# One fused attention and two-MLP kernel on one core: first loads cut and reordered, weight and value splits moved, y stores issued by another engine

## Chip, core and metric

The kernel runs on one core of one Trainium2 chip. The metric is the device time of one execution in microseconds (us). The engines of a core run side by side and meet only at semaphores: TensorE (PE, matmuls and their weight loads), VectorE (DVE), ScalarE (ACT), GpSimd (POOL) and SyncE (SP, which here only issues DMAs). ACT can issue DMAs too. Each engine takes its instructions strictly in the order in which they are written.

## What is computed

Chunked attention with memory keys, then two MLPs on its output; everything in float32.

```python
for c in range(nc):                      # 24 chunks of 32 queries, 16 keys left, 8 right, 8 memory keys
    scores = scale * np.matmul(q_c, k_full.transpose(0, 1, 3, 2))
    scores = scores - np.max(scores, axis=-1, keepdims=True)
    a = np.exp(scores)
    a = a / (np.sum(a, axis=-1, keepdims=True) + 1e-09)
    out[:, :, c_start:c_end] = np.matmul(a, v_full)
x = out.transpose(0, 2, 1, 3).reshape(3072, 512)
h = x @ w_in                             # 512 x 2048
g = np.maximum(h, 0.0) + alpha * np.minimum(h, 0.0)
y = g @ w_out                            # 2048 x 512
return ((y @ w_a) * (y @ w_b)) @ w_out2  # 512 x 1536, 1536 x 512
```

## The kernel before

**Precision by splits.** Matmuls run on operands that are split in two: `hi` is the value rounded to a short float32 form (an ACT copy, helpers `hi_*`), `lo` is the value minus `hi` (a subtraction on POOL or DVE, helpers `lo_*`, `split_*`). A product is three matmuls: hi*hi, hi*lo, lo*hi (lines 585 to 587).

**Tiles.** The 3072 tokens are 8 tiles of 384 tokens. A tile has 8 attention heads; one head of one tile is a *unit*, and comes as one packed array of 128 rows x 1152 columns (K, then Q, each with its 64 rows written twice, then V in columns V0 = 896 and up): 576 KB. Two units make a pair, and a pair gives one quarter of the tile's `x`.

**Prologue (heads 0 to 8).** Units 0 to 10 are loaded into `u_early` by SP. For each head PE computes scores from unsplit data (`score_early`, line 621, into the one bank `s_ps`), DVE masks them and takes the maximum (`softmax_max`, line 1157), ACT takes the exponentials (`exps`, line 897, four per head), DVE inverts the sums, POOL normalises (line 538), PE transposes (line 636), DVE copies the transpose (`copy_pt`, line 1179), and per half pair PE multiplies with V (`mix_early`, line 647), ACT and DVE split the result into `x_hi` (line 915) and `x_lo` (line 1193). Between these stand steps that tile 0 will need: the splits of four weight blocks (`hi_w` on ACT line 886, `lo_w` on POOL line 532; `w_in_prologue(u)` says behind which head's exponentials), of the V of units 8 and 9 (`hi_v` line 872, `lo_v` line 506) and of K and Q of unit 9 (`hi_kq` line 863, `lo_kq` lines 517 and 522). `keep_busy(n)` (line 611) issues n matmuls whose result nobody reads. The first four weight blocks are staged in two slots `w_raw`, so that blocks 2 and 3 are loaded only when blocks 0 and 1 have been split.

**Tiles.** In tile t, for j = 0 to 15, PE computes `up` (12 matmuls, into `h_ps`) for j and `down` (12 matmuls, into four banks) for j - 1, and between them the attention steps of tile t + 1. In tile 0 the weights are split on the way: `up(0, j)` waits for weight block 2j, `down` for block 2j + 1. `up(0, 0)` waits for `x_lo` quarter by quarter; in its middle stand two `keep_busy` matmuls and the last pair's `mix_early`. POOL does per unit `lo_v`, `lo_kq` and, in tile 0, two `lo_w` per j. At the start of tile t + 1 ACT and DVE empty the four banks of tile t into `y_stage`, and ACT issues the store of it to `y_dram` (`store_y`, line 943).

**Second part.** Products of the second MLP (lines 591 to 593) and the last projection (lines 826 to 828), whose 24 outputs ACT copies to `o_stage` (line 1083) and SP stores (line 462).

## Time and profile before

| | us |
|---|---|
| three runs | 1212.30, 1212.31, 1212.92 |
| median | 1212.31 |
| the profiled execution | 1212.38 |
| span of its instructions | 1210.6 |
| PE busy | 1199.2 |
| DVE, ACT, POOL busy | 724.5, 569.0, 256.1 |
| TensorE clock granted, mean | 1.0 of full |

The span is the time from the first to the last instruction or transfer of the profiled execution; 1.8 us of its time lie around it. All times below are us from the start of the span. A row of the timeline has start, duration, engine and line, operation, what it writes and reads, how many were merged, and in brackets how long the engine had been idle and what released it. "PEld" is PE's weight load; "SPq" and "ACTq" are those engines' sequencers issuing DMAs.

### The profile page before, as it was taken

What the parts mean: (1) busy time and instruction counts of PE and PEld (TensorE: products, weight loads), DVE (VectorE), ACT (ScalarE), POOL (GpSimd) and SP (SyncE); (2) the same over time, 40 slices, a digit from 0 to 9 for tenths busy, and PEclk for the clock granted to TensorE, in tenths of its full rate; (3) what the DMA queues carried; (4) which work ended last, traced back from release to release, by engine and by line L of the source; (5) the groups of instructions that cost most, each with busy time, mean ns of one, the idle gap of its engine ahead of it and who ended that gap; (6) DMA issues with size and microseconds to landing.
All of it is one profiled execution on the core that took longest, in us unless ns stands there. A gap on an engine that the chain in (4) does not pass through costs nothing.

```text
span 1210.6 us, 19095 instructions
## 1 busy us (share of the span) xinstructions
PE 1199.2 (99%) x6616; PEld 1094.4 (90%) x6618; DVE 724.5 (60%) x1772; ACT 569.0 (47%) x1404; POOL 256.1 (21%) x234
## 2 busy tenths in 40 slices
PE   8999999999999999999999999999999999999998
PEld 5899999999999999999999888888888888888887
DVE  5777666666666666666555476854475644565421
ACT  6766454545454545454323454543444443444322
POOL 4886232323232323232035000000000000000000
PEclk9999999999999999999999999999999999999999
DMA  7452212112112121121110512022111121111000
GB/s 279 144 164 87 84 60 85 59 59 84 59 58 85 59 84 59 58 85 40 45 53 35 198 37 70 35 96 70 44 35 70 42 98 61 44 40 66 1 35 35
DMA packets 27619, 87.89 MB, mean 73 GB/s; under 512 B 2720, under 2 KB 6816, under 8 KB 25248
## 3 DMA queue, kind: packets, MB, share of 16 engines
q1 hardware_dynamic: 23328, 80.76, 19.9%
q10 hardware_dynamic: 4224, 6.29, 1.4%
q8 instruction: 36, 0.59, 0.2%
q14 instruction: 31, 0.25, 0.1%
HBM read 74.46 MB, written 12.58 MB: 72 GB/s over the span
## 4 chain that ended last, share of the span: by engine, by line
PE 96%; DVE 2%; ACT 1%; DMA 1%; issue 1%; POOL 0%; ACTq 0%; DVEq 0%; POOLq 0%
PE bank L585 16%; PE bank L587 15%; PE bank L586 15%; PE bank L592 9%; PE bank L593 9%; PE bank L591 9%; PE bank L827 5%; PE bank L826 5%; PE bank L828 5%; PE bank L604 2%; PE bank L636 1%; PE bank L603 1%; DMA w_raw<-w 1%; DVE g_lo L1213 0%; PE bank L611 0%
## 5 line engine op out<-in xcount | busy, mean ns | idle before, releaser
L592 PE MATMUL bank<-yc,ws 128*128 128x512 f32 x504 | 196.1, 389 | 0.0
L593 PE MATMUL bank<-yc,ws 128*128 128x512 f32 x504 | 196.1, 389 | 0.0
L591 PE MATMUL bank<-yc,ws 128*128 128x512 f32 x504 | 196.1, 389 | 0.0
L1203 DVE TENSOR_SCALAR g_neg<-bank,al 128x384 f32<-128x384 f32 x128 | 79.0, 617 | 173.8 <-PE bank L587 173.7
L926 ACT ACTIVATE g_hi<-g_raw 128x384 fp32r<-128x384 f32 x128 | 67.2, 525 | 120.3 <-DVE g_raw L1208 120.2
L897 ACT ACTIVATE prob<-prob,neg_max 96x128 f32<-96x128 f32 x220 | 85.7, 391 | 74.9 <-DVE neg_max L1157 74.9
L591 PEld LDWEIGHTS bank<-yc,ws 128*128 128x128 f32 x504 | 94.6, 188 | 19.7
L593 PEld LDWEIGHTS bank<-yc,ws 128*128 128x128 f32 x504 | 94.6, 188 | 19.6
L592 PEld LDWEIGHTS bank<-yc,ws 128*128 128x128 f32 x504 | 94.6, 188 | 19.6
L1402 DVE TENSOR_TENSOR p_split<-p_all,p_split 128x512 fp32r<-128x512 f32 x72 | 49.5, 691 | 93.5 <-ACT p_split L1077 93.4
L1077 ACT ACTIVATE p_split<-p_all 128x512 fp32r<-128x512 f32 x72 | 45.2, 631 | 110.3 <-PE bank L828 100.7
L522 POOL TENSOR_TENSOR k_lo<-u_raw,kq_hi 128x512 fp32r<-128x512 f32 x53 | 68.5, 1293 | 115.9 <-PE bank L604 115.3
L585 PE MATMUL bank<-g_hi,w_first 128*128 128x384 f32 x256 | 88.2, 345 | 0.7 <-DVE g_lo L1213 0.7
L585 PE MATMUL bank<-g_hi,w_later 128*128 128x384 f32 x256 | 88.0, 344 | 0.5 <-DVE g_lo L1213 0.5
L585 PE MATMUL bank<-x_hi,w_first 128*128 (+1 forms) x256 | 87.0, 340 | 1.2 <-DVE x_lo L1193 1.2
L1213 DVE TENSOR_TENSOR g_lo<-g_raw,g_hi 128x384 fp32r<-128x384 f32 x128 | 77.2, 603 | 16.3 <-ACT g_hi L926 12.7
L506 POOL TENSOR_TENSOR v_lo<-u_raw,v_hi 128x256 fp32r<-128x256 f32 x53 | 43.9, 829 | 201.1 <-ACT v_hi L872 201.1
L585 PE MATMUL bank<-x_hi,w_later 128*128 (+1 forms) x256 | 86.4, 338 | 0.0
L587 PE MATMUL bank<-g_hi,w_later 128*128 128x384 f32 x256 | 85.9, 335 | 0.0
L587 PE MATMUL bank<-g_hi,w_first 128*128 128x384 f32 x256 | 85.9, 335 | 0.0
L586 PE MATMUL bank<-g_lo,w_first 128*128 128x384 f32 x256 | 85.8, 335 | 0.0
L586 PE MATMUL bank<-g_lo,w_later 128*128 128x384 f32 x256 | 85.8, 335 | 0.0
(149 smaller groups left out, 3004.1 us busy)
## 6 DMA issues: line engine op xcount, KB each, us to landing
u_raw<-units SPq DMA_DIRECT2D x53, 576.0 KB, 3.7
wr<-w_ab SPq DMA_DIRECT2D x18, 1024.0 KB, 4.8
u_early<-units SPq DMA_DIRECT2D x11, 576.0 KB, 8.9
y_dram<-y_stage ACTq DMA_DIRECT2D x8, 768.0 KB, 4.1
out<-o_stage SPq DMA_DIRECT2D x24, 256.0 KB, 2.0
w_raw<-w SPq DMA_DIRECT2D x16, 256.0 KB, 2.9
y_stage<-w SPq DMA_DIRECT2D x16, 256.0 KB, 3.0
wr<-y_dram SPq DMA_DIRECT2D x8, 512.0 KB, 4.2
```

What stands on the lines that cost most here:

```text
L522: nc.gpsimd.tensor_tensor(k_lo[:, :], src[:, 0:Q0], kq_hi[:, b, 0:Q0].bitcast(F32), ALU.subtract).then_inc(k_lo_done, 1)
L585: nc.tensor.matmul(out_ap, w_hi, m_hi, start=first, stop=False)
L586: nc.tensor.matmul(out_ap, w_hi, m_lo, start=False, stop=False)
L587: return nc.tensor.matmul(out_ap, w_lo, m_hi, start=False, stop=last)
L591: nc.tensor.matmul(out_ap, w_hi, m_hi, start=first, stop=False, skip_group_check=True)
L592: nc.tensor.matmul(out_ap, w_hi, m_lo, start=False, stop=False, skip_group_check=True)
L593: return nc.tensor.matmul(out_ap, w_lo, m_hi, start=False, stop=True, skip_group_check=True)
L826: nc.tensor.matmul(r_ps[u % 2][:, :], hi, w[:, 0], start=g == order[0] and c == 0, stop=False)
L897: last = nc.scalar.activation(dst[:, i, :], src[:, i, :], ACT.Exp, bias=neg_max[:, b, i:i + 1], scale=-1.0, accum_out=row_sum[:, b, i, 0:1])
L926: nc.scalar.activation(g_hi[:, j % 2], g_raw[:, :], ACT.Copy).then_inc(g_hi_done, 1)
L1203: nc.vector.tensor_scalar(g_neg[:, :], h_ps[:, 0:TOK], 0.0, al[:, j:j + 1], ALU.min, ALU.mult)\
L1213: nc.vector.tensor_tensor(g_lo[:, j % 2], g_raw[:, :], g_hi[:, j % 2].bitcast(F32), ALU.subtract)\
```

## The change

Seven edits, all but the last two in the prologue.

1. Of unit 0 only 64 rows and columns 0 to 895 are loaded at first (224 KB), and the scores of head 0 contract over 64 rows with the whole scale; the V columns follow after unit 1 in a load of their own (128 KB).
2. The loads are in another order: weight blocks 0, 1 and 2 stand between units 1 and 4, alpha and block 3 behind unit 8. Each of the four blocks is loaded into the place of its own lower half (`w_first_raw`), so none waits for a slot.
3. The splits of weight blocks 0, 1, 2 follow heads 0, 1, 3 (were 0, 2, 5); block 3 and the V of units 8 and 9 and K, Q of unit 9 come behind the exponentials of head 8 on ACT, and on POOL behind the normalisation of head 8.
4. `keep_busy` has 8 for 10 matmuls at first, 2 for 3 ahead of transposes, and its two in the middle of `up(0, 0)` are gone.
5. The last pair's `mix_early` stands ahead of `up(0, 0)`, not in its middle.
6. The stores of `y` of tiles 0 to 5 are issued by SP, at the head of each pass of its loop, ahead of that tile's unit loads; those of tiles 6 and 7 stay on ACT.
7. The last output block is copied and stored in two halves of 256 columns: the first by SP, the second by ACT.

Core of the diff (declarations of the new semaphores and of `w_first_raw`, and the branches that pick them, are left out):

```diff
@@ sync
+            sp.dma_start(u_early[0:HEAD_DIM, 0, 0:V0], units[0][0:HEAD_DIM, 0:V0]).then_inc(first_loaded, 16)
+            load_early(1)
+            sp.dma_start(u_early[:, 0, V0:], units[0][:, V0:]).then_inc(early_loaded[0], 16)
+            load_w(0)
+            load_early(2)
+            load_w(1)
+            load_early(3)
+            load_w(2)
+            for u in range(4, HEADS + 1):
+                load_early(u)
+            sp.dma_start(al[:, :], alpha).then_inc(alpha_loaded, 16)
+            load_w(3)
...
+            def store_y(t):
+                sp.wait_ge(y_act_done, t + 1)
+                sp.wait_ge(y_dve_done, t + 1)
+                sp.dma_start(y_dram[:, :, bass.ds(t * TOK, TOK)], y_stage[:, :, :]).then_inc(y_stored, 16)
+
             with sp.Fori(1, TILES - 2) as t:
+                store_y(t - 1)
                 for c in range(HEADS):
                     load_unit((t + 1) * HEADS + (c + 4), c % 2)
+            store_y(TILES - 3)
@@ gpsimd
-            return {0: (0,), 2: (1,), 5: (2,), 8: (3,)}.get(u, ())
+            return {0: (0,), 1: (1,), 3: (2,)}.get(u, ())
...
-                if u == 4:
-                    lo_v(HEADS, HEADS)
-                if u == 6:
-                    lo_v(HEADS + 1, HEADS + 1)
-            pool.wait_ge(w_lo_done, W_PROLOGUE)
-            pool.wait_ge(v_lo_done, 2)
+            pool.wait_ge(prob_done, HEADS + 1)
             lo_kq(HEADS + 1, HEADS + 1)
+            lo_w(W_PROLOGUE - 1)
+            lo_v(HEADS, HEADS)
+            lo_v(HEADS + 1, HEADS + 1)
@@ tensor
-                    if first_tile and j == 0 and kt == 2:
-                        keep_busy(2)
-                        mix_early(PAIRS - 1, 0)
-                        mix_early(PAIRS - 1, 1)
...
-            keep_busy(10)
+            keep_busy(8)
...
-                        keep_busy(3)
+                        keep_busy(2)
...
+            mix_early(PAIRS - 1, 0)
+            mix_early(PAIRS - 1, 1)
             tile(0, 2)
@@ scalar
-                    if p == 0 and not first:
-                        store_y(t - 1)
...
-                if u == 3:
-                    hi_v(HEADS, HEADS)
-                if u == 5:
-                    hi_v(HEADS + 1, HEADS + 1)
-                if u == 7:
-                    hi_kq(HEADS + 1, HEADS + 1, 0)
             split_x(PAIRS - 2, 1, PAIRS - 2, 0, True)
+            hi_kq(HEADS + 1, HEADS + 1, 0)
             split_x(PAIRS - 1, 0, PAIRS - 1, 0, True)
             split_x(PAIRS - 1, 1, PAIRS - 1, 0, True)
+            hi_w(W_PROLOGUE - 1)
+            hi_v(HEADS, HEADS)
+            hi_v(HEADS + 1, HEADS + 1)
...
+                half = slice(0, MODEL if u < SUPERS * SUBS - 1 else MODEL // 2)
+                nc.scalar.activation(o_stage[:, u % 2, half], r_ps[u % 2][:, half], ACT.Copy).then_inc(o_done, 1)
...
+            nc.scalar.activation(o_stage[:, 1, MODEL // 2:], r_ps[1][:, MODEL // 2:], ACT.Copy).then_inc(last_copied, 1)
+            act.wait_ge(last_copied, 1)
+            act.dma_start(out[last_row:last_row + P, MODEL // 2:], o_stage[:, 1, MODEL // 2:]).then_inc(last_stored, 16)
```

On ACT, from the exponentials of head 3 (written to `y_stage`; even heads write `prob`) to those of head 7, the kernel before has:

```order
L897 ACTIVATE y_stage,row_sum<-y_stage,neg_max 96x128 x4
L872 ACTIVATE v_hi<-u_early 128x256
L897 ACTIVATE prob,row_sum<-y_stage,neg_max 96x128 x4
L915 ACTIVATE x_hi<-bank 64x192 x2
L897 ACTIVATE y_stage,row_sum<-y_stage,neg_max 96x128 x4
L915 ACTIVATE x_hi<-bank 64x192 x2
L886 ACTIVATE w_first<-w_raw 128x512
L872 ACTIVATE v_hi<-u_early 128x256
L897 ACTIVATE prob,row_sum<-y_stage,neg_max 96x128 x4
L915 ACTIVATE x_hi<-bank 64x192 x2
L897 ACTIVATE y_stage,row_sum<-y_stage,neg_max 96x128 x4
```

and the changed kernel:

```order
L930 ACTIVATE y_stage,row_sum<-y_stage,neg_max 96x128 x4
L919 ACTIVATE w_first<-w_first_raw 128x512
L930 ACTIVATE prob,row_sum<-y_stage,neg_max 96x128 x4
L948 ACTIVATE x_hi<-bank 64x192 x2
L930 ACTIVATE y_stage,row_sum<-y_stage,neg_max 96x128 x4
L948 ACTIVATE x_hi<-bank 64x192 x2
L930 ACTIVATE prob,row_sum<-y_stage,neg_max 96x128 x4
L948 ACTIVATE x_hi<-bank 64x192 x2
L930 ACTIVATE y_stage,row_sum<-y_stage,neg_max 96x128 x4
```

Both copies of V (`v_hi`) have left this stretch, and the weight block stands two heads earlier. Behind them, from head 7's split of `x` to the start of tile 0, the kernel before has on ACT:

```order
L915 ACTIVATE x_hi<-bank 64x192 x2
L863 ACTIVATE kq_hi<-u_early 128x896
L897 ACTIVATE prob,row_sum<-y_stage,neg_max 96x128 x4
L915 ACTIVATE x_hi<-bank 64x192 x2
L886 ACTIVATE w_first<-w_raw 128x512
L915 ACTIVATE x_hi<-bank 64x192 x6
L863 ACTIVATE kq_hi<-u_early 128x896
L872 ACTIVATE v_hi<-u_early 128x256
```

and the changed kernel:

```order
L948 ACTIVATE x_hi<-bank 64x192 x2
L930 ACTIVATE prob,row_sum<-y_stage,neg_max 96x128 x4
L948 ACTIVATE x_hi<-bank 64x192 x4
L893 ACTIVATE kq_hi<-u_early 128x896
L948 ACTIVATE x_hi<-bank 64x192 x4
L919 ACTIVATE w_first<-w_first_raw 128x512
L902 ACTIVATE v_hi<-u_early 128x256 x2
L893 ACTIVATE kq_hi<-u_early 128x896
L902 ACTIVATE v_hi<-u_early 128x256
```

The copy of K and Q of unit 9 went from ahead of head 8's exponentials to the middle of the last splits of `x`. On POOL, from the normalisation of head 6 (into `prob`) to the first weight blocks of tile 0, before:

```order
L538 TENSOR_TENSOR prob<-prob,inv_sum 96x512
L506 TENSOR_TENSOR v_lo<-u_early,v_hi 128x256
L538 TENSOR_TENSOR y_stage<-y_stage,inv_sum 96x512
L538 TENSOR_TENSOR prob<-prob,inv_sum 96x512
L532 TENSOR_TENSOR w_first<-w_raw,w_first 128x512
L517 TENSOR_TENSOR kq_hi<-u_early,kq_hi 64x384
L522 TENSOR_TENSOR k_lo<-u_early,kq_hi 128x512
L506 TENSOR_TENSOR v_lo<-u_early,v_hi 128x256
L517 TENSOR_TENSOR kq_hi<-u_early,kq_hi 64x384
L522 TENSOR_TENSOR k_lo<-u_early,kq_hi 128x512
L532 TENSOR_TENSOR w_first<-w_raw,w_first 128x512 x2
```

and changed:

```order
L569 TENSOR_TENSOR prob<-prob,inv_sum 96x512
L569 TENSOR_TENSOR y_stage<-y_stage,inv_sum 96x512
L569 TENSOR_TENSOR prob<-prob,inv_sum 96x512
L548 TENSOR_TENSOR kq_hi<-u_early,kq_hi 64x384
L553 TENSOR_TENSOR k_lo<-u_early,kq_hi 128x512
L563 TENSOR_TENSOR w_first<-w_first_raw,w_first 128x512
L537 TENSOR_TENSOR v_lo<-u_early,v_hi 128x256 x3
L548 TENSOR_TENSOR kq_hi<-u_early,kq_hi 64x384
L553 TENSOR_TENSOR k_lo<-u_early,kq_hi 128x512
L563 TENSOR_TENSOR w_first<-w_raw,w_first 128x512 x2
```

Two `v_lo` more stand between the last normalisation and the first weight blocks of tile 0 (the last row).

## Rows read from the trace of the kernel before

**Rows 1.** Page, part 1: busy time of each engine.

```profile
PE 1199.2 (99%) x6616; PEld 1094.4 (90%) x6618; DVE 724.5 (60%) x1772; ACT 569.0 (47%) x1404; POOL 256.1 (21%) x234
```

**Rows 2.** Timeline of ACT in the prologue: start, duration, engine, operation, idle.

```profile
14.26 0.40 ACT L897 ACTIVATE y_stage<-y_stage,neg_max 96x128 f32<-96x128 f32 x1
...
18.05 0.42 ACT L872 ACTIVATE v_hi<-u_early 128x256 fp32r<-128x256 f32 x1 [2.14 <-DMA u_early<-units]
...
18.37 0.39 ACT L897 ACTIVATE prob<-y_stage,neg_max 96x128 f32<-96x128 f32 x1
...
29.52 0.39 ACT L897 ACTIVATE prob<-y_stage,neg_max 96x128 f32<-96x128 f32 x1
...
30.97 0.19 ACT L897 ACTIVATION_READ_ACCUMULATOR prob<-y_stage,neg_max 96x1 f32 x1
```

**Rows 3.** Timeline of DVE: first maximum of head 6 and of head 7.

```profile
21.51 0.29 DVE L1157 CUSTOM_DVE_ANT_0 y_stage<-bank,mask 96x128 f32<-96x128 f32 x1
...
23.84 0.29 DVE L1157 CUSTOM_DVE_ANT_0 y_stage<-bank,mask 96x128 f32<-96x128 f32 x1
```

**Rows 4.** Timeline of the start: first load, first matmuls, first weight load of scores.

```profile
0.75 0.86 SPq L392 DMA_DIRECT2D u_early<-units  x2
...
0.79 4.42 PE L611 MATMUL bank<-const-bfloat16-1.0 128*128 128x512 bf16 x10 [0.79 <-PEq L1512]
...
4.96 1.20 PEld L621 LDWEIGHTS bank<-u_early 128*96 128x96 f32 x8 [0.66 <-DMA u_early<-units]
```

**Rows 5.** Page, part 6: loads, count, size of one, median us to landing.

```profile
u_raw<-units SPq DMA_DIRECT2D x53, 576.0 KB, 3.7
...
w_raw<-w SPq DMA_DIRECT2D x16, 256.0 KB, 2.9
```

**Rows 6.** Timeline: head 2's transpose; last mixes, splits of x, last quarter of up(0, 0).

```profile
15.59 0.55 PE L636 MATMUL bank<-ident,prob 96*128 96x96 f32 x4 [0.22 <-POOL prob L538]
...
32.09 1.46 PE L647 MATMUL bank<-pt_early,u_early 128*128 128x192 f32 x8
...
33.89 0.66 ACT L915 ACTIVATE x_hi<-bank 64x192 fp32r<-64x192 f32 x2
...
35.50 0.44 PE L585 MATMUL bank<-x_hi,w_first 128*128 128x384 f32 x1 [0.71 <-DVE x_lo L1193]
```

**Rows 7.** Timeline of POOL from head 8 on, and PE's start of up(0, 2).

```profile
32.63 1.27 POOL L532 TENSOR_TENSOR w_first<-w_raw,w_first 128x512 fp32r<-128x512 f32 x1
...
36.29 0.73 POOL L506 TENSOR_TENSOR v_lo<-u_early,v_hi 128x256 fp32r<-128x256 f32 x1
...
37.10 1.00 POOL L517 TENSOR_TENSOR kq_hi<-u_early,kq_hi 64x384 fp32r<-64x384 f32 x1
...
39.44 2.87 POOL L532 TENSOR_TENSOR w_first<-w_raw,w_first 128x512 fp32r<-128x512 f32 x2
44.58 2.54 POOL L532 TENSOR_TENSOR w_first<-y_stage,w_first 128x512 fp32r<-128x512 f32 x2 [2.28 <-ACT w_first L886]
...
42.17 0.33 PE L585 MATMUL bank<-x_hi,w_first 128*128 128x384 f32 x1
```

**Rows 8.** Timeline: y stores on ACT's queue, and what waits near them.

```profile
122.07 3.02 ACTq L943 DMA_DIRECT2D y_dram<-y_stage  x1
...
127.81 0.44 PE L585 MATMUL bank<-g_hi,w_first 128*128 128x384 f32 x1 [0.72 <-DVE g_lo L1213]
...
136.08 0.95 ACT L863 ACTIVATE kq_hi<-u_raw 128x896 fp32r<-128x896 f32 x1
...
607.27 0.56 ACTq L943 DMA_DIRECT2D y_dram<-y_stage  x1
...
611.37 0.53 ACT L926 ACTIVATE g_hi<-g_raw 128x384 fp32r<-128x384 f32 x1 [3.63 <-DVE g_raw L1208]
```

**Rows 9.** Timeline of the end: last output copy and its store.

```profile
1207.48 0.60 ACT L1083 ACTIVATE o_stage<-bank 128x512 f32<-128x512 f32 x1 [6.98 <-PE bank L828]
...
1208.11 0.33 SPq L462 DMA_DIRECT2D out<-o_stage  x1
```

More of the change, by code:

```diff
@@ L153, in attention_mlp_kernel @@
         x_ps, y_ps, z_ps, r_ps = (s_ps, pt_ps), (o_ps, h_ps), (bank[0], bank[1]), (bank[2], bank[3])
+        first_loaded = sem("first_loaded")
+        w_first_loaded = [sem(f"w_first_loaded{i}") for i in range(W_PROLOGUE)]
         early_loaded = [sem(f"early_loaded{i}") for i in range(EARLY)]
@@ L230, in attention_mlp_kernel @@
         o_done = sem("o_done")
+        last_copied = sem("last_copied")
+        last_stored = sem("last_stored")
         out_stored = [sem(f"out_stored{i}") for i in range(2)]
@@ L257, in stage_of @@
         def stage_of(n):
-            if W_PROLOGUE <= n < W1_UNITS:
-                return (n - W_PROLOGUE) % (W_STAGE + W_MORE)
-            return n % W_STAGE
+            return (n - W_PROLOGUE) % (W_STAGE + W_MORE)
         def w_stage(n):
+            if n < W_PROLOGUE:
+                return w_first_raw[:, n, 1]
             i = stage_of(n)
@@ L267, in before_in_stage @@
         def before_in_stage(n):
-            return [m for m in range(n) if stage_of(m) == stage_of(n)]
+            return [m for m in range(W_PROLOGUE, n) if stage_of(m) == stage_of(n)]
         def parity(t):
@@ L380, in load_w @@
             def load_w(n):
+                if n < W_PROLOGUE:
+                    sp.dma_start(w_stage(n), w1[n]).then_inc(w_first_loaded[n], 16)
+                    return
                 before = before_in_stage(n)
@@ L389, in load_w, with load_early @@
                 sp.dma_start(w_stage(n), w1[n]).then_inc(w_loaded[stage_of(n)], 16)
-            for u in range(EARLY):
+            def load_early(u):
                 sp.dma_start(u_early[:, u], units[u]).then_inc(early_loaded[u], 16)
-                if u == 1:
-                    sp.dma_start(al[:, :], alpha).then_inc(alpha_loaded, 16)
-                    load_w(0)
-                    load_w(1)
+            sp.dma_start(u_early[0:HEAD_DIM, 0, 0:V0], units[0][0:HEAD_DIM, 0:V0]).then_inc(first_loaded, 16)
[10 more added lines that the diff above has]
+            load_w(3)
+            for u in range(HEADS + 1, EARLY):
+                load_early(u)
             load_unit(EARLY, EARLY % 2)
-            for n in range(W_STAGE, W_PROLOGUE + W_STAGE + W_MORE):
+            for n in range(W_PROLOGUE, W_PROLOGUE + W_STAGE + W_MORE):
                 load_w(n)
@@ L461, in store_out @@
                 row = (u // SUBS) * TOK2 + rows_of(u % SUBS) * P
-                sp.dma_start(out[row:row + P, :], o_stage[:, u % 2]).then_inc(out_stored[u % 2], 16)
+                half = slice(0, MODEL if u < SUPERS * SUBS - 1 else MODEL // 2)
+                sp.dma_start(out[row:row + P, half], o_stage[:, u % 2, half]).then_inc(out_stored[u % 2], 16)
             sp.wait_ge(x_lo_done, UNITS)
@@ L486, in _ @@
                 sp.wait_ge(out_stored[i], 16 * SUPERS * SUBS // 2)
+            sp.wait_ge(last_stored, 16)
         @block.gpsimd
@@ L613, in score_early @@
             def score_early(u):
-                pe.wait_ge(early_loaded[u], 16)
+                rows = slice(0, P if u else HEAD_DIM)
+                pe.wait_ge(early_loaded[u] if u else first_loaded, 16)
                 if u:
@@ L618, in score_early @@
                 for i in range(BLOCKS):
-                    q = u_early[:, u, Q0 + i * QB:Q0 + (i + 1) * QB]
+                    q = u_early[rows, u, Q0 + i * QB:Q0 + (i + 1) * QB]
                     at = slice(i * KEYS, (i + 1) * KEYS)
-                    last = nc.tensor.matmul(s_ps[0:QB, at], q, u_early[:, u, at], start=True, stop=True)
+                    last = nc.tensor.matmul(s_ps[0:QB, at], q, u_early[rows, u, at], start=True, stop=True)
                 last.then_inc(scores, 1)
@@ L644, in mix_early @@
                     pe.wait_ge(x_lo_done, (g - 2) * 2 + half + 1)
+                if g == 0 and half == 0:
+                    pe.wait_ge(early_loaded[0], 16)
                 dst = half_bank(g, half, True)
@@ L880, in hi_w @@
             def hi_w(n):
-                act.wait_ge(w_loaded[stage_of(n)], 16 * (len(before_in_stage(n)) + 1))
+                if n < W_PROLOGUE:
+                    act.wait_ge(w_first_loaded[n], 16)
+                else:
+                    act.wait_ge(w_loaded[stage_of(n)], 16 * (len(before_in_stage(n)) + 1))
                 if n == EARLY_SLOTS:
@@ L1082, in empty_o @@
                     act.wait_ge(out_stored[u % 2], 16 * (u // 2))
-                nc.scalar.activation(o_stage[:, u % 2], r_ps[u % 2][:, :], ACT.Copy).then_inc(o_done, 1)
+                half = slice(0, MODEL if u < SUPERS * SUBS - 1 else MODEL // 2)
+                nc.scalar.activation(o_stage[:, u % 2, half], r_ps[u % 2][:, half], ACT.Copy).then_inc(o_done, 1)
             act.wait_ge(x_lo_done, UNITS)
```

10 lines of the change are left out of this document (4 added, 6 removed).

## Prediction, made before the changed kernel ran

> **What bounds the kernel now.** First the busy times: PE is busy 1199.2 us of the 1210.6 us span [rows 1], so only PE's idle time, some 11 us, can be won without less matmul work, and the change takes out only matmuls that nobody reads. The question is therefore where PE idles and whether a moved step opens or closes such a hole. The timeline then shows three places. The first is the prologue, up to the last quarter of up(0, 0) at 35.50 [rows 6]: PE works only in pieces there, and what ends last is the round score, maximum, exponentials, sum, normalise, transpose. The second is one hole of 0.72 us at 127.81 [rows 8]. The third is the end, where nothing but the copy and the store of the last block runs [rows 9]. In the other loop passes PE has no hole at the y stores, so no gain can be had there, only a loss. I work against the profiled execution, 1212.38 us with a span of 1210.6; the median of three, 1212.31, is the same within its scatter (1212.30 to 1212.92). About 0.2%, 2.4 us, is what a measurement of this kernel tells from no change.
>
> **Start of head 0.** Its first weight load is at 4.96, released by the load of unit 0, which SP issued at 0.75: 4.2 us [rows 4]. No row has a load of 224 KB; the nearest are 576 KB in 3.7 us and 256 KB in 2.9 us [rows 5], 0.8 us for 320 KB. The 352 KB fewer give 0.9, so it lands at about 4.05. PE's ten idle-filling matmuls take 4.42 us from 0.79 with their tail, their spacing about 0.43; eight of them end near 4.2. I take 4.25, so 0.7 us sooner. Bounds: 0 if a smaller load lands no sooner, 0.75 where the eight matmuls end. The order of the next loads does not take this back: units 1 to 3 have 0.35, 0.5 and 0.2 MB less ahead of them, units 4 to 8 the same bytes within 0.05 MB. From the landings of units 0 and 8 (4.96, 18.05, with 5.2 MB between them) a unit takes 1.5 us, so unit 4 lands near 12.1 and unit 8 near 18.1; the scores of a head start with the exponentials of the one before, now at 13.55 for head 4 and about 22.9 for head 8, so even the closest has 1.4 us.
> The Trainium skill (DMA: Bandwidth & Descriptors, Rules for kernel authors) advises against two transfers to disjoint partition halves, since both run on the same 16 DMA engines. Here the second 64 rows are not needed at all, but if the rule held for the one half as well, the 0.7 us would be gone and the sum 0.7 us smaller.
>
> **Pace of the heads.** Exponentials of head 3 start at 14.26, then ACT waits for unit 8's landing to copy its V at 18.05, and head 4 starts at 18.37 [rows 2], 1.9 us behind a pace of 2.2 to 2.3. A second loss lies before head 6, where ACT waits for weight block 2 and copies the V of unit 9, a third before head 8: the copy of K and Q of unit 9, 0.95 us as that at 136.08 [rows 8]. Head 8 starts at 29.52 and ends at 31.16 (30.97 + 0.19). With these gone, what is late next? DVE: between maximum of head 6 and of head 7 it works without a gap on maximum, inverse, copy of a transpose and x_lo, 23.84 - 21.51 = 2.33 us [rows 3]. ACT needs less, 1.55 for four exponentials and 0.66 for x_hi. So from head 3, now at 14.26 - 0.7 = 13.55, five steps of 2.33 give head 8 at 25.2 and its end at 26.85, against 31.16: 4.3 us. The weight copies of 0.6 us now stand behind heads 0, 1 and 3, where ACT still has 0.5 us of air a head; I expect at most 0.1 from them, and as much from POOL's block 1 (1.27 us) ahead of head 2's normalisation.
>
> **From head 8 to the tile.** Before, 4.3 us pass from the end of head 8 (31.16) to the last x_lo, and PE starts the last quarter at 35.50 [rows 2, 6]. Now another strand is as long. Head 7's transpose follows head 8's exponentials by 1.35 us (as head 2's at 15.59 follows head 3's at 14.26): 26.55; transpose and its copy 1.15, to 27.7; the last four mixes 1.5 with their start, to 29.3 [rows 6]. On ACT, x_hi of the third pair, then K and Q of unit 9 (0.95) to 29.4, then two x_hi of 0.66 each, to 30.75; x_lo of the last one 0.75, to 31.5. With semaphores I put PE's start at 31.65 for 35.50: **3.85 us sooner**, 0.45 of the 4.3 given back. Bounds 2.9 (DVE pace 2.5 a head) to 4.5 (2.2 a head).
>
> **What the moved splits cost POOL.** Before, the V splits (0.73 each) and block 3 (1.27) lay in POOL's waiting time [rows 7]. Now they stand between head 8 and tile 0. Head 8 normalised: before 32.63, 1.47 behind its exponentials; now DVE's copy at 27.7 holds back the inverse, so 29.25. Then K and Q of unit 9 (from 37.10 to 39.44 such a pair takes 2.34) from 29.45 to 31.8, block 3 to 33.1, three V of 0.8 to 35.45, K and Q of unit 10 to 37.8, weight block 4 of 1.27 to 1.44 to 39.15. up(0, 2) wants that block: it began at 42.17, now 42.17 - 3.85 = 38.3. **PE waits 0.9 us**. Bounds 0.3 to 1.6. Before, POOL had the block ready about 1.3 us early (39.44 + 1.43 = 40.87). The lag does not go on: POOL stood idle for 2.28 us behind block 5, until 44.58, waiting for ACT's copy of block 6, and that idle time takes up the lag. ACT's own three extra copies behind the exponentials (1.6 us with K and Q) end at 33.1, and the transpose it then splits comes at about 33.2, so they are hidden, by 0.1 us only; without that cover up(0, 1)'s follower would be 0.3 late.
>
> **Filler matmuls and the mixes ahead of up(0, 0)** cost nothing: PE waits in both places for x_lo.
>
> **Stores of y.** The first on ACT holds its queue for 3.02 us (122.07), the later ones 0.56 [rows 8]; ACT's next copy of K and Q starts 2.25 late, and in its wake PE stands 0.72 us for g_lo at 127.81. With SP issuing it, that hole closes: **-0.7 us**, bounds 0 and 0.75. The slow first use, if it belongs to ACT's queue, moves to 607.27; ACT idles there from 607.8 until 611.34, so 3.02 us end at 610.3 and stay hidden with 1 us to spare. What is queued behind the new wait on SP are the unit loads. The first of a pass would go out at about 122.6, behind the store, and if it takes 3.7 us after a store that takes 4.9 (a third more), it lands at 131.2; ACT wants it at 136.08 [rows 5, 8]. Hidden with 5 us to spare, in each pass.
>
> **The last store.** Before: copy 1207.48 to 1208.08, issue at 1208.11, end at 1210.6 [rows 9]. Now half copies of about 0.4 (V, as wide, 0.42 [rows 2]) end at 1207.9 and 1208.2; ACT waits for itself and issues at 1208.25, 0.14 later than SP did, with an issue of 0.33 (as SP) to 0.56 (as ACT's earlier ones), but half the bytes behind it (0.4 us less at the rate of rows 5). **-0.1 us**, bounds -0.4 and +0.4.
> The Trainium skill (same page, same section) says that spreading DMAs over SP and ACT saves only issue time and no bandwidth; by it the first half gains nothing and the last term is 0 rather than -0.1.
>
> **Sum.** -3.85 + 0.9 - 0.7 - 0.1 = -3.75, of which 0.7 is the start of head 0. Span 1206.85, time **1208.6 us**. PE stays busy behind tile 0, so what is won early reaches the end.
>
> **Rivals.** (a) The first load does not land sooner, or another load is late: 1209.3 to 1209.4. For it: 4.2 us before is more than the 3.7 of a lone unit, so part is not size. Against it: bytes do count in rows 5. (b) POOL's lag is not taken up: 2.3 us at up(0, 2) and the following blocks instead of 0.9, so 1210.0. For it: POOL is the fullest engine next to PE in tile 0. (c) ACT's first store to the output is slow again, as 122.07 was: the end is 2.5 us later, 1211.1. For it: the row does not say whether the 3.02 us belong to the first use of the queue or of a tensor by it. Against it: the stores at 607.27 and later are other instructions and took 0.56. (d) With fewer fillers TensorE's clock is at 1.2 GHz for part of the prologue or the first matmuls of tile 0. The last mixes take 1.46 us [rows 6] and would cost that much more; the twelve matmuls of up(0, 0), 384 columns at 2.4 GHz or 0.16 us each, 1.9 more: between 1.5 and 3.4, I take 2.1, so 1210.7. Against it: the fillers that go stood where PE now has shorter holes than before.  The Trainium skill (TensorE: Matmul & The Clock Gate, What's actually happening) has the clock follow how busy PE has been and says that the same kernel's start varies; that is this rival. (e) **Slower than before**: SP's wait for the emptied banks holds back unit loads so long that K and Q come late, in all six passes that store from SP. It decides once a pass loses (3.75 + 2.4) / 6 = 1.0 us, that is, when the load lands 6 us later than I worked out; then 1215. (f) Better: POOL runs its row quicker, PE waits 0.3 at up(0, 2) and small holes of 0.2 to 0.25 us in tile 0 close: 1207.5.
>
> **Chances.** Forecast 0.50, (a) 0.14, (b) 0.09, (c) 0.07, (d) 0.05, (e) 0.03, (f) 0.12. Faster by over 0.2% (under 1209.9): forecast, (a), (f), 0.76. Within: (b), (c), (d), 0.21. Slower 0.03. The range 1207.0 to 1210.8 takes in all but (c) and (e), and with the bounds of each term some of the forecast's own tails.
>
> **What the new profile would show.** First score weight load at 4.2 to 4.4; exponentials of head 4 at 15.8 to 16.2 with no wait for a DMA, of head 8 at 25 to 25.6; last quarter of up(0, 0) at 31.3 to 32; a wait of PE for a weight block of POOL ahead of up(0, 2) of about 0.9; no hole near 123 to 124; ACT's store at about 603 of 3 us with no PE hole behind it. Wrong, if PE idles at the head of later tiles, if exponentials wait for `early_loaded`, or if the last store ends more than 3 us behind the last matmul.

## The result, and the profile after

The changed kernel takes 1209.01 us in the median of eight runs (1208.66 to 1210.56), the kernel before on the same chip 1212.4 (1212.15 to 1213.28): a ratio of 0.9972, 95% interval 0.9961 to 0.9983. That is 3.4 us or 0.28%, just over the 0.2% that can be told from no change. The profiled execution took 1208.68, with a span of 1206.9 for 1210.6. From here on, line numbers in rows are those of the kernel that the row belongs to.

Page of the changed kernel, part 1, which answers to [rows 1]: PE's busy time is 1.9 us less, with five idle-filling matmuls fewer, and its idle time 1.8 us less.

```profile
PE 1197.3 (99%) x6611; PEld 1093.2 (91%) x6611; DVE 722.7 (60%) x1772; ACT 568.8 (47%) x1405; POOL 257.0 (21%) x234
```

Timeline of PE in the changed kernel: the start, head 7's transpose, the three holes of over 0.2 us between there and 70 us, and its last matmul (start, duration, operation, count, idle time and what ended it). The rows answer to [rows 4], [rows 6] and [rows 7].

```profile
0.79 3.57 PE L640 MATMUL bank<-const-bfloat16-1.0 128*128 128x512 bf16 x8 [0.79 <-PEq L1541]
4.29 1.25 PE L651 MATMUL bank<-u_early 64*96 64x128 f32 x8
5.47 1.05 PE L640 MATMUL bank<-const-bfloat16-1.0 128*128 128x512 bf16 x4
...
26.32 0.55 PE L666 MATMUL bank<-ident,y_stage 96*128 96x96 f32 x4 [0.67 <-POOL y_stage L569]
...
31.47 0.44 PE L614 MATMUL bank<-x_hi,w_first 128*128 128x384 f32 x1 [0.82 <-DVE x_lo L1223]
...
39.70 0.41 PE L614 MATMUL bank<-x_hi,w_first 128*128 128x384 f32 x1 [1.62 <-POOL w_first L563]
...
62.77 0.44 PE L614 MATMUL bank<-g_hi,w_first 128*128 128x384 f32 x1 [0.25 <-DVE g_lo L1243]
...
1203.50 0.39 PE L858 MATMUL bank<-wo_tail,p_split 128*128 128x512 f32 x1
```

The last quarter of up(0, 0) comes at 31.47 for 35.50: 4.03 us won. Up(0, 2) starts at 39.70 for 42.17: 2.47 left, since PE now waits 1.62 us there. From there the difference is -2.9 at about 55 us (before had a small hole of 0.18 there) and -2.6 behind the 0.25 at 62.77, and it stays so until 124 us; behind the place of the old hole at 127.81 it is 3.56 and stays 3.56 up to the last matmul (1203.50 for 1207.06).

Timeline of ACT in the changed kernel, first exponentials of heads 3, 4 and 8, against [rows 2]:

```profile
13.27 0.40 ACT L930 ACTIVATE y_stage<-y_stage,neg_max 96x128 f32<-96x128 f32 x1 [0.55 <-DVE neg_max L1187]
...
15.47 0.40 ACT L930 ACTIVATE prob<-y_stage,neg_max 96x128 f32<-96x128 f32 x1
...
25.03 0.40 ACT L930 ACTIVATE prob<-y_stage,neg_max 96x128 f32<-96x128 f32 x1
```

Head 4 follows head 3 after 2.20 us (4.11 before) and waits for no load. Head 8 starts at 25.03 for 29.52.

Timelines of POOL and DVE in the changed kernel, the splits behind head 8 up to weight block 4, against [rows 7]:

```profile
31.68 1.28 POOL L563 TENSOR_TENSOR w_first<-w_first_raw,w_first 128x512 fp32r<-128x512 f32 x1
32.94 2.44 POOL L537 TENSOR_TENSOR v_lo<-u_early,v_hi 128x256 fp32r<-128x256 f32 x3
...
36.54 1.30 POOL L553 TENSOR_TENSOR k_lo<-u_early,kq_hi 128x512 fp32r<-128x512 f32 x1
37.80 1.75 POOL L563 TENSOR_TENSOR w_first<-w_raw,w_first 128x512 fp32r<-128x512 f32 x1
...
38.89 1.07 DVE L1243 TENSOR_TENSOR g_lo<-g_raw,g_hi 128x384 fp32r<-128x384 f32 x1 [0.47 <-ACT g_hi L959]
```

POOL's chain stood where it was forecast, within 0.2 us, up to block 4 at 37.80. Block 4 itself took 1.75 us, where block 3 took 1.28. Behind it POOL worked on without a pause until 49.4 us; before, it had stood idle for 2.28 us ahead of 44.58 [rows 7]. The last row is the neighbour that comes back below: a DVE subtraction with two operands in on-chip memory.

Timelines of SP and ACT in the changed kernel at the first store of y, and of ACT at its own first store, against [rows 8]:

```profile
119.23 0.65 SPq L433 DMA_DIRECT2D y_dram<-y_stage  x1
...
120.35 0.94 ACT L893 ACTIVATE kq_hi<-u_raw 128x896 fp32r<-128x896 f32 x1
...
603.71 0.66 ACTq L972 DMA_DIRECT2D y_dram<-y_stage  x1
```

SP issues the store in 0.65 us, ACT's copy of K and Q no longer waits, and no hole stands near 124. ACT's first store, now at 603.71, took 0.66 us and not 3.

Timeline of the end, against [rows 9]:

```profile
1204.20 0.38 ACT L1169 ACTIVATE o_stage<-bank 128x256 f32<-128x256 f32 x1
1204.34 0.33 SPq L492 DMA_DIRECT2D out<-o_stage  x1
1204.61 0.36 ACTq L1171 DMA_DIRECT2D out<-o_stage  x1
```

From the last matmul's start to the end of the span it is 3.4 us for 3.54.

### The profile page after: what moved, and what is told of

The parts are those of the page before. It is cut to its first block, busy times and chain, and to the rows that moved or that the text cites. A ratio compares the mean times of both kernels' runs of the same rounds, so it can differ in the third digit from the quotient of the medians.

```text
span 1206.9 us, 19092 instructions
## 1 busy us (share of the span) xinstructions
PE 1197.3 (99%) x6611; PEld 1093.2 (91%) x6611; DVE 722.7 (60%) x1772; ACT 568.8 (47%) x1405; POOL 257.0 (21%) x234
## 4 chain that ended last, share of the span: by engine, by line
PE 96%; DVE 2%; POOL 1%; issue 0%; ACT 0%; POOLq 0%; DVEq 0%
PE bank L614 16%; PE bank L616 15%; PE bank L615 15%; PE bank L622 9%; PE bank L620 9%; PE bank L621 9%; PE bank L858 5%; PE bank L857 5%; PE bank L856 5%; PE bank L666 2%; PE bank L633 2%; PE bank L632 1%; POOL w_first L563 0%; DVE y_stage L1187 0%; DVE prob L1203 0%
## 5 line engine op out<-in xcount | busy, mean ns | idle before, releaser
L615 PE MATMUL bank<-x_lo,w_first 128*128 (+1 forms) x256 | 85.7, 335 | 0.0
```

The costliest lines, as they stand in the source:

```text
L615: nc.tensor.matmul(out_ap, w_hi, m_lo, start=False, stop=False)
```

## The experiments

The theory: four parts pay, (i) head 0 starts sooner, (ii) the V splits of units 8 and 9 no longer make the exponentials wait for a load, (iii) the y stores leave ACT, (iv) the end; and one part costs, POOL's lag at up(0, 2). The rivals are named run by run. Where a kernel ran only once, spans and rows are compared, not medians.

**The y stores.** First the changed kernel with the stores on ACT again:

```diff
@@ sync, loop
-                store_y(t - 1)
...
-            store_y(TILES - 3)
@@ scalar, pass of a tile
+                    if p == 0 and not first:
+                        store_y(t - 1)
```

> The changed kernel with the loop's y stores issued by ACT again; all else stays. My theory, that the slow first issue on ACT (3.02 us at 122.07 in the kernel before) made the hole of PE: it is slow again, near 119, PE has a hole of about 1 us at 124 to 125, and the span is 0.7 to 1.0 us over the changed kernel's 1206.9. Rival, that the hole came from the phase of tile 1 against tile 0 and went with the prologue: no hole or one under 0.3, span within 0.2 of 1206.9.

Timelines of ACT and PE of this run:

```profile
119.71 3.10 ACTq L969 DMA_DIRECT2D y_dram<-y_stage  x1
...
123.01 0.95 ACT L886 ACTIVATE kq_hi<-u_raw 128x896 fp32r<-128x896 f32 x1 [2.34 <-issue]
...
125.54 0.44 PE L607 MATMUL bank<-g_hi,w_first 128*128 128x384 f32 x1 [0.81 <-DVE g_lo L1242]
```

The 3 us, the late copy and the hole are all back. The span is 1208.2 for 1206.9, 1.3 us more; 0.2 of them already stood just ahead of the hole (a transpose at 124.23 for 124.02), so the store on ACT costs 1.1, a little more than the 0.7 to 1.0 expected. Then the reverse, the kernel before with this one edit:

```diff
@@ sync, loop
+                store_y(t - 1)
...
+            store_y(TILES - 3)
@@ scalar, pass of a tile
-                    if p == 0 and not first:
-                        store_y(t - 1)
```

> The kernel before with one part of the change alone: the stores of y inside the loop are issued by SP instead of ScalarE. My theory (the only effect is that ScalarE is no longer held 3.0 us by its first store in the loop, which left TensorE a hole of 0.72 us at 127.81 and moved the tiles behind it): prologue as before to 0.1 us (last quarter of up(0,0) at 35.5), the hole at 127.8 gone, the part of the run up to there unchanged, and span and time 0.7 to 1.1 us under the kernel before. Rival (SP's wait for the last copy of y holds unit loads behind it, and these come late): a wait for a DMA appears on TensorE or on the splitting engines somewhere in tiles 1 to 5, and the gain is under 0.5 us or a loss.

```profile
35.55 0.44 PE L592 MATMUL bank<-x_hi,w_first 128*128 128x384 f32 x1 [0.72 <-DVE x_lo L1194]
```

The prologue is the old one, the hole is gone, the span is 1209.7 for 1210.6. The median of ten runs is 1211.57 for 1212.45, ratio 0.9993 with 0.9983 to 1.0002: by the medians 0.9 us, by the interval alone not to be told from none. The traces carry the point, and the two pairs agree: 0.9 in the kernel before, 1.1 in the changed one. No wait for a late unit load appeared, so the rival (SP's wait holds loads back) falls.

**What the 3 us belong to.** The kernel before, with the small load of alpha issued by ACT at the start, so that the store in the loop is not the queue's first DMA:

```diff
-                    sp.dma_start(al[:, :], alpha).then_inc(alpha_loaded, 16)
...
+            act.dma_start(al[:, :], alpha).then_inc(alpha_loaded, 16)
```

> The kernel before, with its 8 KB load of alpha issued by ACT ahead of the first exponentials instead of by SP. If the 3.02 us belong to the first use of ACT's queue, this issue takes about 3 us (hidden, ACT has nothing to do before 7.5), the first y store near 122 takes 0.56, the hole at 127.8 is gone and the span is about 1209.8. If they belong to the first pass of the loop's store, the alpha issue takes under 0.7, the store at 122 takes 3 us again and the span stays at 1210.6 within 0.2.

Timelines of ACT and PE of this run:

```profile
0.75 0.43 ACTq L985 DMA_DIRECT2D al<-alpha  x1
...
36.77 0.45 PE L584 MATMUL bank<-x_hi,w_first 128*128 128x384 f32 x1 [1.09 <-DVE x_lo L1193]
...
123.12 0.66 ACTq L942 DMA_DIRECT2D y_dram<-y_stage  x1
```

The store in the loop now takes 0.66 us, so its 3.02 was a first use. But the new first use took 0.43, and the changed kernel's first, at 603.71, took 0.66. What is left is that 3 us were seen only where ACT's first DMA is the one in the loop, whose address comes from a register; both others have fixed addresses. Why that is so stays open. The hole at 127.8 closed, but the prologue came 1.27 us late, so the span, 1210.7, shows no gain.

The lateness has two parts. ACT waited 1.19 us for a weight block at 23.75 (0.21 before), and the exponentials of head 8 started at 30.15 for 29.52: 0.63. The rest, 0.64, goes with TensorE's clock. PE had stood idle for 2.14 us ahead of 27.79 (1.16 before), and then its granted clock fell. Stretch from 30 to 32 us of this run (PE busy and count, granted clock, DMA share, GB/s); in the kernel before the clock in it is 1.00:

```profile
30.00:32.00 2.00, 2.00 (x10) 0.50 0.00 0
```

So the weight block and the clock spoil this run as a measure of what the store costs; it shows only where the 3 us fall.

**Head 0's first load.** The changed kernel with unit 0 loaded whole (576 KB) and first, and with PE's waits for it changed to match. The scores of head 0 still contract over 64 rows.

```diff
-            sp.dma_start(u_early[0:HEAD_DIM, 0, 0:V0], units[0][0:HEAD_DIM, 0:V0]).then_inc(first_loaded, 16)
+            load_early(0)
             load_early(1)
-            sp.dma_start(u_early[:, 0, V0:], units[0][:, V0:]).then_inc(early_loaded[0], 16)
```

> The changed kernel with unit 0 loaded whole and first, and its scores over 128 rows (of twice the size, under the same scale as the half: head 0's result is off, nothing else). If size decides the landing: the first weight load of scores goes from 4.25 back to about 4.95, exponentials of head 3 from 13.27 to about 13.95, and the span rises by 0.5 to 0.7. If a later step takes it up (the load of unit 2, for which head 2's scores waited 0.46 us in the changed kernel): the span rises by the part that this load adds, 0.3 to 1.0. If nothing depends on it: within 0.1.

The expectation's words on the scores of head 0 don't fit the kernel as it ran: they contract over 64 rows of real data, and nothing is left out. Timeline of PE:

```profile
4.79 1.29 PE L650 MATMUL bank<-u_early 64*96 64x128 f32 x8 [0.44 <-DMA u_early<-units]
...
32.02 0.44 PE L613 MATMUL bank<-x_hi,w_first 128*128 128x384 f32 x1 [0.83 <-DVE x_lo L1220]
```

Head 0 starts 0.5 us later, the last quarter of up(0, 0) 0.55, and the span is 1207.5 for 1206.9. So the smaller load does land sooner and nothing behind it swallows the gain. Rival (a) falls. The size of the gain is less sure, since the landing itself varies. In the seven traces here where head 0's weight load follows a first load of 224 KB, it starts at 4.29, 4.29, 4.41, 4.42, 4.47, 4.48 and 4.59 us; in the five with 576 KB at 4.76, 4.79, 4.86, 4.89 and 4.96. The medians differ by 0.44 us, and the changed kernel's profiled execution is one of the earliest of its kind, that of the kernel before the latest.

**The V splits.** The changed kernel with the V splits of units 8 and 9 back between the heads, on both engines:

```diff
@@ scalar (gpsimd likewise, one head later)
+                if u == 3:
+                    hi_v(HEADS, HEADS)
+                if u == 5:
+                    hi_v(HEADS + 1, HEADS + 1)
...
-            hi_v(HEADS, HEADS)
-            hi_v(HEADS + 1, HEADS + 1)
```

> The changed kernel with one part undone: the V splits of units 8 and 9 stand again after heads 3 and 5 on ScalarE and after heads 4 and 6 on GpSimd. My theory (the pace of the heads after head 3 was set by ScalarE waiting for unit 8's late landing, which came at about 18 us): ScalarE waits ahead of head 4 again, the exponentials of head 4 begin near 18.4 us instead of 15.5 and those of head 8 near 27.5 to 29 instead of 25.0, the last quarter of up(0,0) comes at 33.5 to 35.5 us instead of 31.5, and GpSimd, freed of the V splits behind head 8, lets up(0,2) wait less than the 1.6 us it waits now; the span is 1 to 3 us above the changed kernel's 1206.9. Rival (the heads are paced by VectorE's maxima anyway, and the landing is hidden): head 8 stays within 0.5 us of 25.0 and the span within 0.5 us of 1206.9 or below it, because up(0,2) waits less.

Timelines of ACT and PE:

```profile
18.65 0.42 ACT L904 ACTIVATE v_hi<-u_early 128x256 fp32r<-128x256 f32 x1 [1.26 <-DMA u_early<-units]
18.97 0.39 ACT L932 ACTIVATE prob<-y_stage,neg_max 96x128 f32<-96x128 f32 x1
...
34.83 0.44 PE L616 MATMUL bank<-x_hi,w_first 128*128 128x384 f32 x1 [1.05 <-DVE x_lo L1227]
```

ACT waits for unit 8's landing again, and every head from 4 on is 3.3 to 3.6 us later; the last quarter is 3.36 later. Up(0, 2) no longer waits, and the span is 1208.4 for 1206.9. Moving these two V splits thus brings 3.4 us at up(0, 0), gives 1.8 back behind it, nearly all at up(0, 2), and 1.5 is left. The rival falls. Head 0's scores took 2.02 us in this execution, for 1.25, and head 3's exponentials started 1.94 us later than in the changed kernel. The wait for unit 8 took all of it up and was still 1.26 us long. This matters for the runs on the clock below. Unit 8 came at 18.65 here and between 17.56 and 18.05 in the versions of the kernel before, which adds to what the splits in this place cost.

**Why POOL is late at up(0, 2).** The changed kernel with weight block 4 split right behind block 3, ahead of the V splits, on ACT and POOL (and issued to match by SP):

```diff
             lo_w(W_PROLOGUE - 1)
+            lo_w(W_PROLOGUE)
@@ scalar
             hi_w(W_PROLOGUE - 1)
+            hi_w(W_PROLOGUE)
```

> The changed kernel with weight block 4 split directly behind block 3, on ACT and on POOL, ahead of the V splits of units 8 to 10. The changed kernel's PE waits 1.62 us for that block ahead of up(0, 2). My theory, that POOL's lag is all of this wait: block 4 is done near 34.3, PE has no hole ahead of up(0, 2) (at most 0.2), and the span falls by 1.0 to 1.6 us, to 1205.3 to 1205.9, about 0.1%. Rival, that the next step is as late (K and Q of unit 10, V of units 8 and 9, or ACT's exponentials): a hole of about the same size opens up to 15 us later and the span falls by under 0.5.

Timelines of PE and POOL:

```profile
6.24 1.89 PE L641 MATMUL bank<-const-bfloat16-1.0 128*128 128x512 bf16 x4
...
33.21 0.44 PE L615 MATMUL bank<-x_hi,w_first 128*128 128x384 f32 x1 [0.80 <-DVE x_lo L1225]
34.66 1.29 POOL L563 TENSOR_TENSOR w_first<-w_raw,w_first 128x512 fp32r<-128x512 f32 x1
...
51.28 0.41 PE L615 MATMUL bank<-x_hi,w_first 128*128 128x384 f32 x1 [0.66 <-POOL w_first L563]
```

Up(0, 2) waits no more, but 0.66 us come back 11 to 12 us later for another block. POOL had no pause up to there, and that block (48.93) took it 2.20 us instead of 1.28 to 1.30, for the reason below. The median is 1208.99 (ratio 0.9962, 0.9948 to 0.9976), with five times in two groups: 1207.2 and 1207.3, and 1209.0 to 1209.5. The profiled execution belongs to the late group, and its first row says why. The four idle-filling matmuls behind head 0 took 1.89 us, for 1.05 in the changed kernel's profiled execution (5.47 above). That is nearly twice the time for the same work, TensorE's 1.2 instead of 2.4 GHz. The granted clock in the views is 1.00 in both stretches, so only the durations show the level. The up(0, 0) of this execution is 1.74 us late by it. Behind tile 0's holes it is only 0.3 later than the changed kernel (124.33 for 124.02), so at an equal clock block 4 in this place is worth 1.4 us; the two early times, 1207.2 and 1207.3 for 1208.7, say the same. So a second question arose: the clock.

The length of block 4 has a partner in the trace before. Timelines of DVE and POOL of the kernel before:

```profile
38.21 1.69 DVE L1213 TENSOR_TENSOR g_lo<-g_raw,g_hi 128x384 fp32r<-128x384 f32 x1
...
39.44 1.61 POOL L532 TENSOR_TENSOR w_first<-w_raw,w_first 128x512 fp32r<-128x512 f32 x1
```

The same `g_lo` takes DVE 0.56 us alone (at 44.02 before) and 1.69 or 1.07 beside POOL's subtraction; a weight block takes POOL 1.28 alone and 1.61 to 2.2 beside DVE's. Not both lose each time: in the run above, POOL's block at 40.78 took 2.22 while `g_lo` beside it, at 41.30, took 0.54. This agrees with the Trainium skill (SBUF — State Buffer, Who interferes with whom): a VectorE instruction with two SBUF inputs contends with a GpSimd instruction that reads SBUF. No run here moved one away from the other alone, so it is argued from rows, not shown by an edit.

**Another place for the V splits.** Block 4 early as above, and the V splits of units 8 and 9 after heads 6 and 7, where both units have landed and POOL has idle time:

```diff
@@ scalar (gpsimd likewise)
+                if u in (HEADS - 2, HEADS - 1):
+                    hi_v(u + 2, u + 2)
...
-            hi_v(HEADS, HEADS)
-            hi_v(HEADS + 1, HEADS + 1)
```

> The changed kernel with weight block 4 split right behind block 3 and with the V splits of units 8 and 9 moved forward again by little: after heads 6 and 7 on both engines, where both units have landed. GpSimd then has its 2.5 us of V splits behind it when it takes up the last normalization. Theory (what is left of GpSimd's lag is made of the V splits behind head 8): the 0.66 us that TensorE waited for a weight block near 51 us with block 4 moved alone is gone, up(0,2) does not wait, ScalarE's exponentials of heads 7 and 8 come up to 0.6 us later; the span is 0 to 0.7 us under that of the kernel with block 4 moved alone, at an equal clock: near 1205.5, or 1207.2 in an execution in which the clock rises late. Rival (ScalarE's two copies, 0.3 to 0.6 us each ahead of exponentials on the critical chain, cost as much as the hole that closes): head 8's exponentials start 0.6 to 1.0 later and the span is equal or up to 0.4 above it.

Timelines of POOL and PE:

```profile
26.22 0.73 POOL L537 TENSOR_TENSOR v_lo<-u_early,v_hi 128x256 fp32r<-128x256 f32 x1
...
31.91 0.44 PE L615 MATMUL bank<-x_hi,w_first 128*128 128x384 f32 x1 [1.26 <-DVE x_lo L1225]
```

Behind 31.91 PE has no hole at up(0, 2), none near 51 and none at 62; up(0, 0) is 0.44 later. -1.62 - 0.25 + 0.44 = -1.43, and the span is 1205.5 for 1206.9. The median of four is 1207.37 (1207.31 to 1207.69), ratio 0.9958 with 0.9941 to 0.9974. So POOL's lag behind head 8 is made of these V splits and the block behind them. But it is not shown to be better than block 4 early alone. Its median is the lowest here because all four of its times lie together; the two early ones of block 4 alone, 1207.22 and 1207.30, are as low. The hole near 51 closed, and ACT's two copies ahead of the exponentials took it back: head 8 starts at 25.66 for 25.03. The rival of the expectation, that they cost as much as they bring, holds for the span.

**The clock at the start.** If the level rises late in some executions, does the kernel before lose by it as well? The theory: its wait for unit 8's landing absorbs it. Both kernels with only four idle-filling matmuls ahead of head 0, so that the lower level is there on purpose (shown for the kernel before; the changed one has 8 there):

```diff
-            keep_busy(10)
+            keep_busy(4)
```

> The kernel before with 4 instead of 10 filler matmuls ahead of head 0, so that TensorE's granted clock is at its lower level for the first heads on purpose. It tests why the changed kernel's times spread by some 1.7 us where those of the kernel before did less. Theory (in the kernel before, head 4's exponentials wait until 18.05 us for unit 8's landing whatever went before, so 1 to 2 us lost in heads 0 to 3 are absorbed there): scores of heads 0 and 1 take 1.7 to 2.1 us instead of 1.1, head 3's exponentials come 1 to 2 us later, head 4's stay within 0.3 us of 18.4, the last quarter of up(0,0) stays within 0.4 us of 35.5, and the span within 0.4 us of 1210.6. Rival (the lateness goes through to the end): last quarter and span 1 to 2 us later.

```profile
4.86 2.02 PE L621 MATMUL bank<-u_early 128*96 128x128 f32 x8 [2.21 <-DMA u_early<-units]
...
8.19 1.03 PE L621 MATMUL bank<-u_early 128*96 128x128 f32 x8
...
17.77 0.42 ACT L872 ACTIVATE v_hi<-u_early 128x256 fp32r<-128x256 f32 x1 [1.32 <-DMA u_early<-units]
...
35.29 0.45 PE L585 MATMUL bank<-x_hi,w_first 128*128 128x384 f32 x1 [0.72 <-DVE x_lo L1193]
```

> The changed kernel with 4 instead of 8 filler matmuls ahead of head 0, the partner of the run on the kernel before. Theory (behind the change no landing gates the heads any more, so what the clock costs heads 0 to 2 goes through): scores of heads 0 and 1 take 1.7 to 2.1 us, head 3's and head 8's exponentials are both 1.3 to 2.5 us later than the 13.3 and 25.0 of the changed kernel, and the last quarter of up(0,0) as much after 31.5; part of it is given back at up(0,2), where TensorE waits 1.6 us for GpSimd, if GpSimd's chain is then no later by the same amount; it is fed by the same heads, so I expect none back: span 1208.2 to 1209.4, times in one group near 1210 to 1211. Rival (the spread of the changed kernel has another cause): span within 0.5 us of 1206.9.

```profile
4.48 2.02 PE L651 MATMUL bank<-u_early 64*96 64x128 f32 x8 [1.83 <-DMA u_early<-units]
...
8.11 1.77 PE L651 MATMUL bank<-u_early 128*96 128x128 f32 x8
...
15.28 0.40 ACT L930 ACTIVATE y_stage<-y_stage,neg_max 96x128 f32<-96x128 f32 x1 [0.55 <-DVE neg_max L1187]
...
33.49 0.44 PE L614 MATMUL bank<-x_hi,w_first 128*128 128x384 f32 x1 [0.80 <-DVE x_lo L1223]
...
41.73 0.41 PE L614 MATMUL bank<-x_hi,w_first 128*128 128x384 f32 x1 [1.60 <-POOL w_first L563]
```

In both, head 0's scores take 2.02 us. In the kernel before, ACT's wait ahead of head 4 shrinks from 2.14 to 1.32 and the last quarter comes at 35.29, not later at all: span 1210.2, median 1212.45 for 1212.66 (ratio 0.9996, 0.9987 to 1.0006). In the changed kernel, head 3 and the last quarter both come 2.0 later, the hole at up(0, 2) is unchanged, span 1209.0 for 1206.9, and all ten times lie at 1210.2 to 1211.0 (ratio 0.9982, 0.9972 to 0.9991). The theory holds: the old wait was a cushion, and with it gone the start's clock goes straight into the time.

The two traces are not an equal trial, though. In the kernel before the level rose ahead of head 1's scores (1.03 us), in the changed kernel only behind them (1.77), so head 3's exponentials came 0.54 us later in the one and 2.01 in the other. That the wait takes up the full amount is seen in the run with the V splits back, where 1.94 were taken up, and the ten times of the kernel before, all within 0.9 us, agree.

The one late time of the changed kernel, 1210.56, lies where a late rise puts it; its trace was not taken. Nor is this the only source of scatter: with its ten fillers the kernel before has late executions of its own, 1212.13 to 1214.23 in the nineteen taken beside these runs. No trace shows one of them, and a cushioned start does not explain them.

Can more work ahead bring the level up reliably? Block 4 early as above, and ten idle-filling matmuls ahead of head 0, three ahead of early transposes:

```diff
-            keep_busy(8)
+            keep_busy(10)
...
-                        keep_busy(2)
+                        keep_busy(3)
```

> The changed kernel with weight block 4 split right behind block 3 and with more filler matmuls in the prologue: 10 instead of 8 ahead of head 0 and 3 instead of 2 at the later place. It asks whether TensorE's granted clock, which in one execution rose only after head 1's scores and in another before head 0's, can be brought up reliably. Theory (more work ahead brings the 2.4 GHz level sooner in every execution): head 0's score matmuls take 1.25 us for the eight, not 2.0, the single times of the rounds lie within 0.5 us of each other, and the median is near 1207.3 to 1208.0, the last since ten fillers end at about 5.2 us and hold head 0 by up to 0.9. Rival (the level's rise does not depend on the fillers): the times still fall in two groups some 1.7 us apart, both later than without the added fillers by the 0.5 to 0.9 us that head 0 starts later; median 1208.0 to 1209.9.

```profile
5.14 2.02 PE L652 MATMUL bank<-u_early 64*96 64x128 f32 x8
...
34.07 0.45 PE L615 MATMUL bank<-x_hi,w_first 128*128 128x384 f32 x1 [0.83 <-DVE x_lo L1225]
```

No: six times from 1207.64 to 1209.92, and in the profiled one head 0's scores still take 2.02 us although 4.4 us of matmuls stand ahead of them. The times did not fall in two clean groups as the rival had it, either. Head 0 starts 0.85 us later for nothing. Median 1208.67 (ratio 0.9965, 0.9952 to 0.9977).

**The last store.** The changed kernel with its last block copied and stored whole:

```diff
-                half = slice(0, MODEL if u < SUPERS * SUBS - 1 else MODEL // 2)
-                sp.dma_start(out[row:row + P, half], o_stage[:, u % 2, half]).then_inc(out_stored[u % 2], 16)
+                sp.dma_start(out[row:row + P, :], o_stage[:, u % 2]).then_inc(out_stored[u % 2], 16)
```

> The changed kernel with its last output row block copied whole by ScalarE's one activation and stored whole (256 KB) by SP, as in the kernel before. Theory (the split of the last store was worth the 0.15 us by which the stretch from the last matmul to the end of the span shortened): that stretch is 3.5 us again instead of 3.4, and the rest as in the changed kernel. Rival (two queues issuing at the same time cost as much as they bring): the stretch stays 3.4 us or gets shorter.

```profile
1203.65 0.39 PE L856 MATMUL bank<-wo_tail,p_split 128*128 128x512 f32 x1
...
1204.70 0.33 SPq L491 DMA_DIRECT2D out<-o_stage  x1
```

From the last matmul to the end of the span 3.55 us (1207.2 - 1203.65), as before the change, for 3.4. So the halves are worth 0.15. It is one profile of each, and the smallest effect here.

## Why the prediction was right, step by step

The forecast was 1208.6 us with a span of 1206.85; measured were 1209.01, and 1208.68 with a span of 1206.9 in the profiled execution. The sum is right partly by luck: POOL's term missed by 0.7 us one way, and the prologue (0.2), the stores (0.3) and small changes of PE's holes in tile 0 (0.1) the other way. The profiled execution is also an early one, 0.3 us under the median.

- **Start of head 0**: 4.25 forecast, 4.29 measured. Undoing it cost 0.5 to 0.6 rather than 0.7, since the whole unit also landed sooner than [rows 4] had it (4.79 for 4.96); over all traces the difference is 0.44, so this forecast met its number partly through the scatter of the landing.
- **Pace of the heads**: head 8 at 25.2 forecast, 25.03 measured; steps of 2.20 to 2.44 for 2.33. Of the two further losses that I named, before heads 6 and 8, none is left.
- **From head 8 to up(0, 0)**: -3.85 forecast, -4.03 measured. The strand through head 7's transpose (26.32) and the two through ACT and DVE ran as laid out.
- **POOL's moved splits**: the mis-sized term. 0.9 us forecast with bounds 0.3 to 1.6, 1.62 measured, just over the upper bound and halfway to the 2.3 of rival (b). The chain was right up to block 4 at 37.80 for 37.8; but PE was ready 0.2 sooner than I had it, and block 4 took 1.75 where I had counted 1.27 to 1.44. The 1.44 was half of a merged row of two (39.44, 2.87), which hid one of 1.61 and one of 1.27. A long one stands beside DVE's `g_lo`; I had not looked at what DVE does at that time. PE lost nothing more at the following blocks, unlike in rival (b). But the step by which POOL's idle time behind block 5 takes up the lag is off as well: POOL paused only at 49.4 us.
- **y stores**: -0.7 forecast with 0.75 as the bound, 0.98 in the traces of the two kernels (from -2.58 to -3.56), 0.9 in the run of this edit alone, 1.1 where it alone was undone. I priced the hole at 127.81 and not what small delays ACT's late copy left around it. That the slow first use moves to ACT's next store was wrong: it is gone.
- **Last store**: -0.1 forecast, -0.15 measured.
- **Rival (d), the clock**: I gave it 0.05 and tied it to the matmuls that the change takes out. It happens, in several executions of these versions, and costs 1.7 to 2.0 us, but not, as far as shown, for that reason: with ten ahead of head 0 and three ahead of early transposes again it still happens. What the change does is take away the wait that hid it.
- Rivals (a), (c), (e), (f) did not occur.

One by one, V splits 1.5, head 0's load 0.6, y stores 0.9 to 1.1 and the last store 0.15 make 3.15 to 3.35 of the 3.7 us of span. The moved weight splits and mixes were not tried alone; whether the rest is theirs or scatter between single executions stays open.

## What to carry over

A copy that waits for a late transfer, placed in the stream of the engine that paces a stage, holds the whole stage: put it where its data has landed. Behind everything it piles up on the next engine (here 1.6 us of 3.4 were given back); what won this back was to split the block that PE wants next ahead of the copies. When executions fall in groups, compare like with like: a lower median can be no more than luck with the group. A wait that is removed was also a cushion: ask what varies ahead of it, since that now reaches the end. And read durations one by one, where two operations are merged in a row, beside what the neighbouring engine does at that moment.

## What was not expected of the hardware

- ACT's first DMA took 3.02 and 3.10 us where it was the one in the loop with an address from a register, and 0.43 and 0.66 us where it had a fixed address. After an early one, the one in the loop took 0.66.
- Behind the same eight 512-column matmuls (3.57 us, in two kernels with the same matmuls up to there), four more took 1.05 us in one execution and 1.89 in another: either level of TensorE's clock, with the granted clock given as 1.00 in both. Ten instead of eight ahead did not settle it.
- Behind 2.14 us without work PE's granted clock was 0.50 from 30 to 32 us in one run.
- DVE's subtraction of 128x384 took 0.56 us alone and up to 1.69 beside one on POOL, whose own went from 1.28 to 1.61, 1.75 and 2.2. Which of the two is held, and for how long, differed each time.
